# Gate logits of a mixture layer: eight gate columns held in the array, x moving, in three column groups

## The reference, cut to what matters

```python
x = attention(q, k, v)                  # 1536 tokens, 512 wide
x = (h * sigmoid(h)) @ w_out            # h = x @ w_in, d_ff 2048
logits = x @ w_gate                     # (1536, 512) @ (512, 8)
logits = logits - logits.max()
P = np.exp(logits)
for _ in range(8):
    P /= P.sum(1, keepdims=True) + 1e-09
    P /= P.sum(0, keepdims=True) + 1e-09
    P *= N / E
for e in range(8):
    out += P[:, e:e + 1] * (np.maximum(x @ w1[e], 0.0) @ w2[e])
```

## Time and profile before

| what | value |
|---|---|
| median of 3 runs | 1427.76 us (1427.58 to 1427.85) |
| the profiled execution's own time | 1426.06 us |
| its span | 1424.3 us |
| TensorE busy | 98% of the span |
| VectorE busy | 56% |
| ScalarE busy | 44% |
| GpSimd busy | 23% |
| share of the chain that ended last on TensorE | 84% |
| granted TensorE clock, mean | 0.991 |

### The profile page before, as it was taken

How to read it: one execution, slowest core, us unless ns; L and a number is a source line. 1 busy time by engine, 2 the same in 40 slices (tenths; PEclk the granted TensorE clock), 3 DMA queues, 4 the chain that set the end, 5 groups by cost and what they waited for, 6 DMA issues and landing times.

```text
span 1424.3 us, 19942 instructions
## 1 busy us (share of the span) xinstructions
PE 1390.7 (98%) x7345; PEld 1275.9 (90%) x7345; DVE 803.3 (56%) x1458; ACT 624.1 (44%) x1316; POOL 321.3 (23%) x391
## 2 busy tenths in 40 slices
PE   6999899999999999999999999999999999999998
PEld 5887899999998799898989989798998989899897
DVE  5565848665727664554646445664645546464452
ACT  5676526343415253442625335362533426253350
POOL 7130221330301220303022030402203030230200
PEclk9999999999979999999999999999999999999999
DMA  8310221221201221212222121322222122221211
GB/s 193 91 32 18 78 84 49 82 89 35 78 27 52 67 75 60 89 45 75 65 69 79 55 89 45 100 74 79 74 60 89 45 74 68 66 85 49 75 30 59
DMA packets 64786, 97.88 MB, mean 69 GB/s; under 512 B 18608, under 2 KB 33968, under 8 KB 64688
## 3 DMA queue, kind: packets, MB, share of 16 engines
q1 hardware_dynamic: 64688, 96.57, 22.7%
HBM read 93.41 MB, written 3.15 MB: 68 GB/s over the span
## 4 chain that ended last, share of the span: by engine, by line
PE 84%; DVE 8%; POOL 2%; ACT 2%; issue 1%; DMA 1%; ACTq 0%; SPq 0%; DVEq 0%; POOLq 0%
PE bank L654 37%; PE bank L719 34%; PE bank L716 6%; PE bank L563 2%; DVE up_l L1186 2%; PE bank L527 2%; PE bank L738 1%; POOL up_raw L461 1%; DVE hid_l L1233 1%; PE bank L540 1%; DVE hid_h L1231 1%; ACT parts L939 1%; DMA up_raw<-w_up 1%; DVE parts L1202 1%; DVE xc_l L1209 1%
## 5 line engine op out<-in xcount | busy, mean ns | idle before, releaser
L654 PE MATMUL bank<-xc_h,up_h 128*128 128x384 f32 x1120 | 378.8, 338 | 6.4 <-ACT bank L928 3.5
L654 PE MATMUL bank<-xc_h,up_l 128*128 128x384 f32 x1120 | 376.7, 336 | 0.0
L654 PE MATMUL bank<-xc_l,up_h 128*128 128x384 f32 x1120 | 376.5, 336 | 0.0
L719 PE MATMUL bank<-down_h,hid_h 128*128 128x512 f32 x768 | 300.2, 391 | 1.9 <-DVE down_l L1191 1.9
L719 PE MATMUL bank<-down_l,hid_h 128*128 128x512 f32 x768 | 300.3, 391 | 0.0
L719 PE MATMUL bank<-down_h,hid_l 128*128 128x512 f32 x768 | 300.2, 391 | 0.0
L461 POOL TENSOR_TENSOR up_raw<-up_raw 128x256 f32<-128x256 f32 x80 | 78.1, 976 | 929.4 <-DMA up_raw<-w_up 929.4
L1186 DVE TENSOR_TENSOR up_l<-up_raw,up_h 128x512 fp32r<-128x512 f32 (+1 forms) x240 | 203.5, 882 | 61.6 <-ACT up_h L868 61.3
L654 PEld LDWEIGHTS bank<-xc_h,up_h 128*128 128x128 f32 x1120 | 211.6, 189 | 12.9 <-issue 5.2
L654 PEld LDWEIGHTS bank<-xc_l,up_h 128*128 128x128 f32 x1120 | 211.6, 189 | 3.1 <-issue 0.2
L654 PEld LDWEIGHTS bank<-xc_h,up_l 128*128 128x128 f32 x1120 | 211.5, 189 | 0.0
(11 more groups left out here) (114 smaller groups left out, 1596.6 us busy)
## 6 DMA issues: line engine op xcount, KB each, us to landing
up_raw<-w_up SPq DMA_DIRECT2D x80, 512.0 KB, 3.7
down_raw<-w_down SPq DMA_DIRECT2D x160, 256.0 KB, 2.7
q_sb<-qT SPq DMA_DIRECT2D x12, 256.0 KB, 4.0
k_sb<-kT SPq DMA_DIRECT2D x24, 128.0 KB, 4.1
v_sb<-v SPq DMA_DIRECT2D x24, 128.0 KB, 3.8
out<-x_sb SPq DMA_DIRECT2D x12, 256.0 KB, 2.6
vg_sb<-v SPq DMA_DIRECT2D x16, 4.0 KB, 1.9
nraw<-n_global SPq DMA_DIRECT2D x1, 1.0 KB, 2.5
```

What stands on the lines that cost most here:

```text
L654: mm = nc.tensor.matmul(ps[:, 0:HALF], a[quad % UP_BUFS][:, w, k, :], b[x][:, k, :], start=(n == 0 and not add), stop=(n == 5), skip_group ...
L719: mm = nc.tensor.matmul(ps[:], x[a][:, t // 3, t % 3 * P:t % 3 * P + P], w[b], start=start, stop=stop)
```

## The change

The operands of the logits change places. The gate's eight columns are loaded, and 512 tokens of x move past them. Three blocks of 512 tokens go to three groups of 32 columns of the array, so that their results stand on partitions 0 to 7, 32 to 39 and 64 to 71 of `g_ps`; the loop over the four blocks of features is the outer one. The result has experts on partitions and tokens along the row. ScalarE copies its 72 partitions to SBUF (`keep_logits`, ahead of `keep_p1` of quad 1, into a part of `parts` that expert steps leave unused), and TensorE turns it back in four float32 products with columns of the identity (`turn_logits`, between P5 and P4 of quad 1). The order of token blocks within `mix` becomes another (`mix_of`).

What stands behind it moves. `turn_top` goes behind P6 instead of ahead of P4, `spread_top` behind P3 instead of ahead of it, `exp_gate` behind `keep_u3` instead of behind `keep_u2`, `rows_even` to the head of quad 2, `token_sums(0)` between P4 and P6 of quad 2 instead of behind P7 of quad 1, and `round_on(0)` behind `hidden21` instead of ahead of it. `top_logit(0)`, `(1)` and `(2)` go behind `hidden22`, `hidden11` and `hidden12`. The rounds from `token_sums(1)` on keep their places.

```diff
+        WIDE = 4
+        TB = NT // WIDE
+        LOGITS = 32 * (TB - 1) + E
+        def mix_of(t):
+            return t % WIDE * TB + t // WIDE
+        def logits_kept():
+            return parts[0:LOGITS, V11:V11 + 2, :].rearrange("p a b -> p (a b)")[:, 0:WIDE * P]
...
-                    for t in range(NT):
-                        for k in range(KT):
-                            mm = nc.tensor.matmul(g_ps[:, t * E:(t + 1) * E], x_sb[:, k, t * P:(t + 1) * P], gate_sb[:, k, :],
-                                                  start=(k == 0), stop=(k == KT - 1))
+                    for k in range(KT):
+                        for t in range(TB):
+                            mm = nc.tensor.matmul(g_ps[32 * t:32 * t + E, :], gate_sb[:, k, :],
+                                                  x_sb[:, k, t * WIDE * P:(t + 1) * WIDE * P],
+                                                  start=(k == 0), stop=(k == KT - 1), skip_group_check=True)
...
+                def turn_logits():
+                    pe.wait_ge(gate_kept, 1)
+                    place = ident[0:LOGITS, 0:32 * TB].rearrange("p (b r) -> p b r", r=32)[:, :, 0:E]
+                    for n in range(WIDE):
+                        mm = nc.tensor.matmul(g_ps[:, n * TB * E:(n + 1) * TB * E], logits_kept()[:, n * P:(n + 1) * P], place,
+                                              start=True, stop=True)
...
                         if s == GATE and i == 1:
-                            turn_top()
+                            turn_logits()
                         if i > 0:
                             p4(s * FP + i - 1)
+                        if s == GATE and i == 2:
+                            token_sums(0)
                         if s > 0 or i > 0:
                             p6(s, i)
+                        if s == GATE and i == 1:
+                            turn_top()
                         p2(s, i)
+                        p3(s, i)
                         if s == GATE and i == 1:
                             spread_top()
-                        p3(s, i)
                         p7(s, i)
                         if s == GATE and i == 0:
                             logits()
-                        elif s == GATE:
+                        elif s == GATE and i > 1:
                             token_sums(i - 1)
...
+                def keep_logits():
+                    act.wait_ge(gate_done, 1)
+                    nc.scalar.copy(logits_kept(), g_ps[0:LOGITS, :]).then_inc(gate_kept, 1)
...
-                            weight = mix[:, c * QB + t, e:e + 1]
+                            weight = mix[:, mix_of(c * QB + t), e:e + 1]
```

More of the change, by code:

```diff
@@ L194, in mixture_kernel @@
         gate_done = sem("gate_done")
+        gate_kept = sem("gate_kept")
         gate_step = sem("gate_step")
@@ L735, in logits @@
                     pe.wait_ge(acc_ready, outs_before[GATE])
-                    for t in range(NT):
-                        for k in range(KT):
-                            mm = nc.tensor.matmul(g_ps[:, t * E:(t + 1) * E], x_sb[:, k, t * P:(t + 1) * P], gate_sb[:, k, :],
-                                                  start=(k == 0), stop=(k == KT - 1))
+                    for k in range(KT):
[3 more added lines that the diff above has]
+                                                  start=(k == 0), stop=(k == KT - 1), skip_group_check=True)
+                    mm.then_inc(gate_done, 1)
+                def turn_logits():
[4 more added lines that the diff above has]
+                                              start=True, stop=True)
                     mm.then_inc(gate_done, 1)
@@ L964, in quad_work @@
                     first = s == 0 and i == 0
+                    if s == GATE and i == 1:
+                        keep_logits()
                     if not first:
@@ L980, in quad_work @@
                     keep_u2(s, i)
-                    if s == GATE and i == 1:
-                        exp_gate()
                     hidden11(s, i)
@@ L993, in quad_work @@
                     keep_u3(s, i)
+                    if s == GATE and i == 1:
+                        exp_gate()
                     if i == 2:
@@ L1255, in top_logit @@
                 def top_logit(step):
-                    dve.wait_ge(gate_done, step + 1)
+                    dve.wait_ge(gate_done, step + 2)
                     if step == 0:
@@ L1287, in quad_work @@
                     gate = s == GATE and i == 1
-                    if gate:
-                        top_logit(0)
+                    if s == GATE and i == 2:
+                        dve.wait_ge(gate_exp, 1)
+                        rows_even()
                     if i > 0:
@@ L1292, in quad_work @@
                     if gate:
-                        top_logit(1)
-                    if s == GATE and i >= 2:
-                        round_on(i - 2)
+                        top_logit(0)
+                    if s == GATE and i == 3:
+                        round_on(1)
                     if i > 0:
                         hidden21(s, i - 1)
+                    if s == GATE and i == 2:
+                        round_on(0)
                     if i == 2:
@@ L1304, in quad_work @@
                         split_down(s * FT + 2 * i)
-                    if gate:
-                        top_logit(2)
                     hidden11(s, i)
                     if gate:
-                        dve.wait_ge(gate_exp, 1)
-                        rows_even()
+                        top_logit(1)
                     if i == 2:
@@ L1321, in quad_work @@
                     hidden12(s, i)
+                    if gate:
+                        top_logit(2)
                     add22(s, i)
```

## The result

| | before | changed |
|---|---|---|
| median of 5 runs | 1427.58 us (1421.40 to 1427.85) | 1411.47 us (1409.79 to 1414.03) |
| ratio | | 0.9901, 95% interval 0.9886 to 0.9916 |
| profiled execution, span | 1426.06, 1424.3 us | 1410.81, 1409.1 us |

The kernel became faster, by 1.0% (0.84 to 1.14). Against the 1427.76 us that the prediction started from, the ratio is 1413.6 us, 14.1 less, where 11.7 were forecast.

What follows compares the result with a forecast made beforehand. TensorE, with a matmul in flight for 98% of the span, was taken as the bound. Terms summed to 8.7 us instead of 20.4, 11.7 less than the 1427.76 us median: 1416.0 us, range 1412.5 to 1422.5.

Steps and rivals of the forecast that it cites:

- The base: First L738 start to quad 2: 27.72 us less 7.28 for the same products leaves 20.44 us of gate cost, all replaced.
- the case that I took: New logits on TensorE: column-group matmuls overlap two at a time, 13 slots; 6.0 us, time 1416.0, chance 0.36.
- a rival with a chance of 0.18: New logits: all three column groups run side by side; logits 3.8 us, time 1413.8, chance 0.18.
- The logits' term: 24 new logit matmuls: 13 slots of 0.435 us plus 0.3 for changes of shape, 6.0 us, between 3.8 and 10.7.
- if starts keep the order of issue: Step for the logit matmuls: a waiting second half holds back later groups, so two run at a time, 5.65 us.
- The loads: New logits' operand loads: covered by the matmul before, cost nothing; rival with them exposed 2.6 us, time 1418.6, chance 0.06.
- The clock: At the new logits: upper level expected; rivals with it falling, 1419.9 with overlap, 1429.3 without, chance 0.07 each.
- Later waits: Quad 3, P5 and P6 may wait because round_on(0) follows hidden21; 0.2 us, between 0 and 0.5.
- The stretch at half clock at 474.30: Behind a wait of the rounds: moving everything earlier may remove or double this stretch, 1.6 us either way.

Runs made afterwards that it cites:

- e1: Changed kernel with the 24 logit matmuls reordered, column groups in the outer loop, eight of one group in a row; the piece took 6.98 us, 16 slots.
- e9: Changed kernel with the logit matmuls reordered: for two feature blocks at a time, four matmuls of each group in turn; 8 slots.
- e2: Changed kernel with all three token blocks sent to column group 0, overwriting each other; the 24 matmuls took 10.40 us, 24 slots.
- e4: Changed kernel with the same logits computed four times over, 96 matmuls of 512 columns; 13.84 us for 32 slots.
- e5: The changed kernel run once more, unaltered, as yardstick; 1413.05 us, ratio 0.9907 to the kernel before.
- e6: Changed kernel's new logits, with the gate's later steps back in their places of before; 1412.33 us, ratio 0.9912 to the kernel before.
- e10: Changed kernel with the logits as before, no copy or turning back, old block order, later steps in new places; 1425.36 us, ratio 0.999 to before.
- e7: Changed kernel with token_sums(5), (6) and (7) one tile of the down projection later each; 1409.66 us, ratio 0.9888 to the kernel before.
- e8: Changed kernel with the last three token sums later, top_logit(1) ahead of hidden11, and an early one-column exponent on ScalarE; 1408.94 us, ratio 0.9882 to before.

## Why the prediction was right, and where it was off

**The base.** The 20.44 us that the gate cost in its interval held. The changed kernel shows no ordinary matmul at half speed and no L738 there. The time came out inside the range, but not by the case that I took: it came by a rival with a chance of 0.18, which the range took in.

**The logits' term was mis-sized: 6.0 forecast, 3.75 measured.** The price of a slot was right (0.435 from the earlier trace rows, 0.43 measured), and so was 0.3 us for entering and leaving: 3.75 less 8 x 0.43 is 0.3. What failed is the step "if starts keep the order of issue". e1 and e9 show that they do not: a group's matmul passes those that wait for another group, so both passes of a product can follow each other without cost, and the first rival, all three side by side, is the case that came. It was priced at 1413.8 with a chance of 0.18; the ratio gives 1413.6.

**The loads** were covered, as I took them to be. A load is in flight for 0.84 of the 3.66 us and the slot is no longer than in the untiled rows. The rule of the Trainium skill, TensorE: Matmul & The Clock Gate, Part 3 (What overlaps and what doesn't), would have added to each slot; this trace does not agree. The three groups stream 10.40 / 3.54 = 2.94 times as fast as one (e2 and the changed kernel's own piece on the chain). The Trainium skill, same page, Part 3 (Measured speedup vs the span model), has 2.38 for three column groups, which is less.

**The clock.** It did not fall, and e2 and e4 show it would not have with one group or with four times the work. The clock is the larger half of the gain. I had named it in the 20.44 us but not sized it: 96 matmuls at 0.107 are 10.3 us, at the clock they were granted they took 16.06, and the ordinary matmuls behind them lost 2.6 more. That is 8.4 of the 14.2 us that the terms come to below.

**`turn_logits`** 0.9 forecast; 411.00 to 412.25 less two slots, 0.90. **`turn_top`** 0.1 forecast; 414.01 to 414.47 less two slots, 0.11. **`spread_top`** 1.0 forecast; 416.23 to 417.46 less two slots, 0.88, with 0.31 idle where I said 0.5, released by VectorE as I said. **`token_sums(0)`** 0.5 forecast; 421.28 to 422.25 less two slots, 0.62. `exp_gate` held `keep_p1` back as worked out, and TensorE did not wait for it. **Later waits**, 0.2 forecast: from the first logit matmul to `token_sums(2)`, at 434.11 after and 447.63 before, is 28.67 against 43.05 us, 14.4 less. The terms with the measured logits (20.44 - 3.75 - 0.9 - 0.1 - 0.9 - 0.6) give 14.2, so nothing was given back there. The ratio's 14.1 us is the same; the 2.4 us beyond the forecast are the logits' 2.25 and this 0.2.

**The stretch at half clock at 474.30** The earlier trace rows is absent from the first profile of the changed kernel (1.6 us more gain there, as priced) and present in e5's (1.7 us less). It is a matter of the run. Ten of the twelve profiles have a TensorE wait of 2.0 to 2.6 us ahead of the last but one of the token sums. In seven of them a stretch of 3.4 us at half clock begins 0.3 to 1.5 us behind it; in three (the changed kernel's first, e6, e10) none does. e7 and e8, without that wait, show none there, but one at 899, behind a wait of 1.86 us. So such a wait is likely to bring it on, in some executions; these counts don't prove it.

## What to carry to other kernels

When a float32 product has few columns on one side, try holding the few and moving the many. Here the slot then cost what the moving columns cost (0.43 us for 512), and the clock's part was the larger gain. Matmuls of different column groups shared a slot, all three of them when at most four of one group followed each other; with eight in a row part of it was lost. So mix the groups in the order of issue. Before arguing about order, run the two orders: the profile settled at once what I had put at 0.36 and 0.18. When a dependent chain (reduce, spread, exponent) is threaded through a busy stream, place each step by the time its input is ready; the moves brought 0.8 us with the new logits (one profile each), and two waits of the rounds that they left alone were worth 3.1 in the gate step. Compare what lies behind the stretch as well: there e7 and e8 lost 1.06 us of it.

## What the runs showed of the hardware that was not expected

- Matmuls to different column groups started out of the order of issue, past three waiting ones of each other group (e1: 16 slots; e9: 8 slots).
- Three float32 matmuls of 512 moving columns in three groups streamed in the 0.43 us of one, for 13.8 us on end (e4).
- Matmuls that load 8 columns and move 512 ran at a granted clock of 1.00 for 10.4 us in one group (e2), where those that load 128 and move 8 were at 0.50 after 4.8 us and after 5.5 us (e10).
- A wait of TensorE of 1.9 to 2.6 us was followed in some executions, within 1.5 us, by 3.4 us at a clock of 0.50, and in others of the same kernel by none: it cost 1.7 us in e5's gate step.
- A one-column exponent in a pause of ScalarE took the table load of 1.28 us there, and the copies and relus after it brought no further load (e8).
